# Attention with a two-layer network behind it: when the tiles of h are split, where their halves lie, and which engine splits them

## What is computed

```python
# attention per (batch, head): scores kept where the hash bits of q and k agree
x = attn_out.transpose(0, 2, 1, 3).reshape(B * S, H * D)     # 1536 x 512
h = np.maximum(np.maximum(x @ w1, x @ w2), x @ w3)           # 1536 x 768
y = h @ w_out                                                # 1536 x 512
u = y @ w_in                                                 # 1536 x 2048
g = u * (1.0 / (1.0 + np.exp(-1.702 * u)))
out = g @ w_out2                                             # 1536 x 512
```

## Time and profile before

| | |
|---|---|
| median of 3 runs | 701.23 us (699.51 to 701.7) |
| the profiled execution: device time | 701.48 us |
| its span, first to last instruction | 699.4 us |
| mean granted clock of PE | 0.989 |
| quads, on PE | end at 372.45 us |
| product with w_out, on PE | 372.45 to 430.29 us |
| second network | 430.29 to the end |

### The profile page before, as it was taken

The page is one execution under the profiler, slowest core; times in us unless marked ns, Lnnn a source line. Parts: engine busy times, 40 slices in busy tenths (PEclk is TensorE's granted clock), DMA queues, the critical chain, the costliest instruction groups (busy, mean ns, idle before and its releaser), DMA issues.

```text
span 699.4 us, 11088 instructions
## 1 busy us (share of the span) xinstructions
PE 684.3 (98%) x3970; PEld 596.6 (85%) x3970; DVE 377.2 (54%) x675; ACT 273.9 (39%) x572; POOL 402.9 (58%) x452
## 2 busy tenths in 40 slices
PE   6999999999999999999997999999999999999998
PEld 4777777777767799999996999999999999999996
DVE  6667676767677799768579512322222242222222
ACT  3777777877777530000005113222222232222222
POOL 4755756688876999878738113344444444444441
PEclk9899999999999999999998999999999999999999
DMA  5835736637341110120010101122222141222202
GB/s 119 200 88 137 169 85 152 160 86 177 96 129 62 31 31 30 31 60 25 23 45 1 61 16 45 48 73 62 73 64 61 45 166 61 60 67 69 65 26 90
DMA packets 67141, 54.07 MB, mean 77 GB/s; under 512 B 29200, under 2 KB 56080, under 8 KB 67088
## 3 DMA queue, kind: packets, MB, share of 16 engines
q1 hardware_dynamic: 66768, 53.36, 28.6%
q10 hardware_dynamic: 320, 0.01, 0.0%
HBM read 32.51 MB, written 3.15 MB: 51 GB/s over the span
## 4 chain that ended last, share of the span: by engine, by line
PE 90%; DVE 7%; DMA 1%; issue 1%; SPq 0%; ACTq 0%; ACT 0%; DVEq 0%
PE psS L1017 10%; PE psR L1025 9%; PE psO L1039 9%; PE psR L1087 8%; PE psR L1085 8%; PE psR L1086 8%; PE psS L1085 5%; PE psS L1086 5%; PE psS L1087 5%; PE psS L1188 4%; PE psS L1189 4%; PE psS L1187 4%; DVE probs L856 2%; PE psR L986 2%; PE psO L1188 1%; PE psO L1187 1%
## 5 line engine op out<-in xcount | busy, mean ns | idle before, releaser
L431 POOL TENSOR_SCALAR w_hi<-w_raw 128x512 fp32r<-128x512 f32 (+2 forms) x134 | 84.6, 634 | 189.0 <-PE psO L1189 129.1
L953 DVE TENSOR_TENSOR probs_t<-psR,probs_t 128x384 f32<-128x384 f32 x64 | 35.7, 557 | 181.9 <-ACT probs_t L748 181.9
L456 POOL TENSOR_SCALAR probs<-probs,inv 128x768 f32<-128x768 f32 x96 | 86.4, 909 | 69.1 <-DVE inv L790 68.2
L748 ACT ACTIVATE probs_t<-psR 128x384 f32<-128x384 f32 x64 | 31.5, 492 | 187.9 <-PE psR L1087 187.9
L779 DVE TENSOR_REDUCE neg_max<-psS 128x1 f32<-128x768 f32 x96 | 91.7, 956 | 21.9 <-PE psS L1017 17.6
L565 POOL TENSOR_TENSOR w_lo<-w_raw,w_hi 128x512 fp32r<-128x512 f32 (+1 forms) x68 | 90.8, 1336 | 5.7
L617 ACT ACTIVATE probs<-psS,neg_max 128x768 f32<-128x768 f32 x96 | 86.4, 900 | 11.7 <-DVE neg_max L779 11.7
L1025 PE MATMUL psR<-ident,probs 128*128 128x128 f32 x576 | 75.2, 275 | 0.7 <-DVE bits L774 0.6
L626 ACT ACTIVATE probs_t<-psR 128x384 f32<-128x384 f32 x128 | 59.4, 490 | 35.2 <-PE psR L1025 35.1
L1025 PEld LDWEIGHTS psR<-ident,probs 128*128 128x128 f32 x576 | 67.4, 142 | 4.7 <-issue 2.1
L1039 PE MATMUL psO<-probs_t,v_raw 128*64 128x384 f32 x384 | 68.8, 494 | 0.0
(11 more groups left out here) (197 smaller groups left out, 1544.7 us busy)
## 6 DMA issues: line engine op xcount, KB each, us to landing
w_raw<-in_moe_w_in SPq DMA_DIRECT2D x32, 256.0 KB, 2.7
w_raw<-in_moe_w_out SPq DMA_DIRECT2D x32, 256.0 KB, 2.6
w_raw<-in_moe_w SPq DMA_DIRECT2D x9, 512.0 KB, 3.8
h_lo<-w_hi SPq DMA_DIRECT2D x22, 192.0 KB, 3.4
h_hi<-w_hi SPq DMA_DIRECT2D x18, 192.0 KB, 3.6
w_raw<-in_q SPq DMA_DIRECT2D x16, 192.0 KB, 3.3
w_raw<-in_k SPq DMA_DIRECT2D x16, 192.0 KB, 3.7
v_raw<-in_v SPq DMA_DIRECT2D x16, 192.0 KB, 2.6
```

The source lines that it names most:

```text
L431: return pool.tensor_scalar(dst, src, 1.0, 1.0, ALU.mult, ALU.mult)
L456: pool.tensor_scalar(probs[i % PROBS][:, :], probs[i % PROBS][:, :], inv[:, i % 6:i % 6 + 1], 1.0, ALU.mult, ALU.mult).then_inc(probs_norm ...
```

## The change

1. **Room.** The six arrays `probs` of the attention are given back after use, and `early_h`, of the same size, takes their place. The split halves of batch 0, f = 0, 1, 2 lie there (`EARLY_H` = 3); f = 3, 4, 5 go to `places` 0 to 5, which are free after quad 14. Batch 1 takes `places` 8 to 15 and two chunks of x.
2. **Three tiles early.** ACT copies and DVE subtracts f = 0, 1, 2 of batch 0 behind quad 5, 7 and 11. The DVE instructions stand after all of the quad's own.
3. **The other three by DVE in the last quad.** Six subtractions of 384 columns stand between quad 15's additions; the maxes 1 to 3 come after them. POOL makes no more subtractions for h.
4. **POOL waits.** Split d = 1 of w_out waits for `h_lo_made` 12, the last subtraction of batch 0.
5. **Batch 1 spread.** ACT copies it in halves behind batch 0, each f as soon as its maxes are done. DVE does three of its 12 subtractions ahead of each of the first four `y_lo`, where it did all 12 ahead of the first.
6. PE's order stays; its waits in the tiles 0, 1 and 8 name the new counts.

```diff
-        probs = [sb(f"probs{i}", [P, S], F32) for i in range(PROBS)]
+        with ExitStack() as attention:
+            probs = [attention.enter_context(nc.sbuf_tensor(f"probs{i}", [P, S], F32)) for i in range(PROBS)]
+
+        early_h = sb("early_h", [P, PROBS, S], F32R)
...
+        EARLY_H = 3
+
         def h_part(b, f, lo):
             if b == 0:
-                return places[2 * f + lo]
-            return places[12 + 2 * f + lo] if f < 2 else (x_hi, x_lo)[lo][:, KC + f - 2, :]
+                return early_h[:, 2 * f + lo, :] if f < EARLY_H else places[2 * (f - EARLY_H) + lo]
+            return places[8 + 2 * f + lo] if f < 4 else (x_hi, x_lo)[lo][:, KC + f - 4, :]
...
+        def hidden_done(b, f):
+
+            return h_maxed, 2 * (B * (f - f % 2) + 2 * b + f % 2 + 1)
+
+        def early_after(n):
+
+            return {5: (0,), 7: (1,), 11: (2,)}[n] if n in (5, 7, 11) else ()
...
                 pool.wait_ge(*used(ALL_PARTS - SLOTS + 3 * d + 2))
+                if d == 1:
+                    pool.wait_ge(h_lo_made, 2 * UPS)
                 split(ts(d, S), w_raw[:, k % 3 * BLOCK_COLS:k % 3 * BLOCK_COLS + S], w_hi_made, w_split, ALL_PARTS + d)
-                if d == 0:
-                    for f in range(4):
-                        pool.wait_ge(h_hi_made, f + 1)
-                        pool.tensor_tensor(h_part(0, f, 1), hidden[0][:, f, :, :].rearrange("p j q -> p (j q)"),
-                                           f32(h_part(0, f, 0)), ALU.subtract).then_inc(h_lo_early, 1)
...
             for n in range(QUADS):
                 copy_part(n)
-
-            act.wait_ge(h_maxed, 4 * B * FPS - 4)
+                for f in early_after(n):
+                    if f == 0:
+                        act.wait_ge(*t_split(1, 4))
+                    for j in range(2):
+                        h_hi(0, f, j)
+
             act.wait_ge(quad_made, 7 * (QUADS - 1))
-            for f in range(4):
-                h_hi(0, f)
+            for j in range(2):
+                for f in range(EARLY_H, UPS):
+                    h_hi(0, f, j)
             act.wait_ge(quad_made, 7 * QUADS)
-            for j in range(2):
-                for f in (4, 5):
-                    h_hi(0, f, j)
-            act.wait_ge(h_maxed, 4 * B * FPS)
             for f in range(UPS):
-                h_hi(1, f)
+                for j in range(2):
+                    h_hi(1, f, j)
...
             for n in range(QUADS):
+                last = n == QUADS - 1
                 add_quad(n, 0)
                 add_quad(n, 1)
                 max_quad(n, 0)
+                if last:
+                    for i in range(6, 9):
+                        h_lo(i)
                 add_quad(n, 2)
                 add_quad(n, 3)
+                if last:
+                    for i in range(9, 12):
+                        h_lo(i)
...
+                for f in early_after(n):
+                    h_lo(2 * f)
+                    h_lo(2 * f + 1)
+            for n in range(2 * OUTS):
+                for i in range(3 * n, 3 * n + 3):
+                    if i < 2 * UPS:
+                        h_lo(2 * UPS + i)
+                y_lo(n)
+            for n in range(2 * OUTS, 2 * OUTS * B):
                 y_lo(n)
...
                 if n == 0:
-                    waits = {0: (h_lo_early, 1), 1: (h_lo_early, 2), 2: (h_lo_early, 3), 3: (h_lo_early, 4),
-                             4: (h_lo_made, 1), 5: (h_lo_made, 2)}
+                    waits = {0: (h_lo_made, 6), 3: (h_lo_made, 7), 4: (h_lo_made, 8), 5: (h_lo_made, 9)}
                 elif n == 1:
-                    waits = {4: (h_lo_made, 3), 5: (h_lo_made, 4)}
+                    waits = {3: (h_lo_made, 10), 4: (h_lo_made, 11), 5: (h_lo_made, 12)}
                 elif n == 2 * OUTS:
-                    waits = {f: (h_lo_made, 6 + 2 * f) for f in range(UPS)}
+                    waits = {f: (h_lo_made, 2 * UPS + 2 * f + 2) for f in range(UPS)}
```

More of the change, by code:

```diff
@@ L235, in lsh_attention_ffn @@
         h_lo_made = sem("h_lo_made")
-        h_lo_early = sem("h_lo_early")
         y_ready = sem("y_ready")
@@ L712, in copy_part, with h_hi @@
                 act.activation(quad_parts[n % 2][0], product_bank(7 * n), ACT.Copy).then_inc(part_copied, 1)
[L714 to L717, removed]
+            def h_hi(b, f, j):
+                if j == 0:
+                    act.wait_ge(*hidden_done(b, f))
+                act.activation(h_part(b, f, 0)[:, ts(j, HALF)], hidden[b][:, f, j, :], ACT.Copy).then_inc(h_hi_made, 1)
             for n in range(QUADS):
                 copy_part(n)
-            act.wait_ge(h_maxed, 4 * B * FPS - 4)
+                for f in early_after(n):
[3 more added lines that the diff above has]
+                        h_hi(0, f, j)
             act.wait_ge(quad_made, 7 * (QUADS - 1))
-            for f in range(4):
-                h_hi(0, f)
+            for j in range(2):
+                for f in range(EARLY_H, UPS):
+                    h_hi(0, f, j)
             act.wait_ge(quad_made, 7 * QUADS)
-            for j in range(2):
-                for f in (4, 5):
-                    h_hi(0, f, j)
-            act.wait_ge(h_maxed, 4 * B * FPS)
             for f in range(UPS):
-                h_hi(1, f)
+                for j in range(2):
+                    h_hi(1, f, j)
             def y_hi(n):
@@ L914, in max_quad, with h_lo, y_lo @@
                     mx.then_inc(h_maxed, 1)
-            def h_lo(n, b, f, j):
+            h_order = [(0, f, j) for f in range(EARLY_H) for j in range(2)]
+            h_order += [(0, f, j) for j in range(2) for f in range(EARLY_H, UPS)]
+            h_order += [(1, f, j) for f in range(UPS) for j in range(2)]
+            def h_lo(n):
+                b, f, j = h_order[n]
                 cols = ts(j, HALF)
-                dve.wait_ge(h_hi_made, n)
+                dve.wait_ge(h_hi_made, n + 1)
                 dve.tensor_tensor(h_part(b, f, 1)[:, cols], hidden[b][:, f, j, :], f32(h_part(b, f, 0)[:, cols]),
                                   ALU.subtract).then_inc(h_lo_made, 1)
+            def y_lo(n):
+                b, d, j = n // (2 * OUTS), n // 2 % OUTS, n % 2
+                dve.wait_ge(y_hi_made, n + 1)
+                dve.tensor_tensor(y_part(b, d, 1)[:, ts(j, HALF)], psY[n % len(psY)][:, 0:HALF],
+                                  f32(y_part(b, d, 0)[:, ts(j, HALF)]), ALU.subtract).then_inc(y_lo_made, 1)
             for n in range(QUADS):
+                last = n == QUADS - 1
                 add_quad(n, 0)
@@ L933, in _ @@
                 max_quad(n, 3)
[L934 to L939, removed]
-            def y_lo(n):
-                b, d, j = n // (2 * OUTS), n // 2 % OUTS, n % 2
-                dve.wait_ge(y_hi_made, n + 1)
-                dve.tensor_tensor(y_part(b, d, 1)[:, ts(j, HALF)], psY[n % len(psY)][:, 0:HALF],
-                                  f32(y_part(b, d, 0)[:, ts(j, HALF)]), ALU.subtract).then_inc(y_lo_made, 1)
-            for n in range(2 * OUTS * B):
+                for f in early_after(n):
[7 more added lines that the diff above has]
+            for n in range(2 * OUTS, 2 * OUTS * B):
                 y_lo(n)
```

## The result

The changed kernel takes 692.89 us (median of 4 runs, 692.58 to 693.41) where the kernel before took 701.32 (699.51 to 701.7; four runs, where the table of before has three): a ratio of 0.9886, with a 95% interval of 0.9867 to 0.9904, or 8.4 us less. Measured again beside e9 it was 693.72 against 701.48, ratio 0.9891 [0.9869, 0.9914]. The forecast was 693.8, in a range of 692.2 to 696.4.

A forecast was written before the change was run, and what follows sets the result against it. PE, busy 98% of the span, was taken as the bound, so only its waits or lower clock could be won. In the w_out stage 7.85 us removed less 0.15 put back gives 7.7: 701.48 - 7.7 = 693.8 us, range 692.2 to 696.4.

The forecast's parts named there:

- The last quad and tile 0: Start of the w_out stage: batch 0's last subtraction ends at 374.5, so tile 0's 6.67 us of waits go.
- POOL's wait is hidden: Split d = 1 of w_out, held for h_lo_made 12, is still done 1.0 us before PE's tile 2 wants it.
- The tie at the first y_lo: Tile 4 of w_out: y_lo ends at 384.95, needed at 384.93; 0 to 0.5 us of stall, 0.15 taken.
- The granted clock stays at 1.00: w_out stage: PE no longer pauses, so its clock does not fall and that part of the 1.18 us goes.
- list of losses: w_out stage's 7.92 us lost: 6.67 before tile 1, 1.18 up to tile 4 (clock and first y_lo), 0.07 after.
- The early splits cost nothing: Splits behind quads 5, 7, 11: lag 0.94 to 2.98 us against 1.36 slack at quad 7; none taken, at most 1.6.
- rival B: Early splits of quad 7 press on PE, up to 1.6 us of stall: 695.4 us; chance 0.10.
- The total: Whole kernel: 701.48 less 7.7 gives 693.8 us, range 692.2 to 696.4.
- A: POOL keeps DVE out without turns, PE stalls at tile 3 of w_out, some 2.8 us: 696.4 us; chance 0.07.
- C: No change: DVE's queue is so long that the first y_lo still comes at 392: 701 us; chance 0.03.
- D: DVE becomes the bound of all quads, eight quads with maxes lose 10.4 us: 704.2 us; chance 0.04.

The follow-up runs named there:

- e9: Changed kernel with POOL waiting for h_lo_made 9 and tiles f = 0 and 1 both split behind quad 5, none behind quad 7: 694.16 us, ratio 0.9902.
- e1: Changed kernel without POOL's wait for h_lo_made 12 before split d = 1 of w_out: stage 51.73 us, total 693.73 us.
- e6: Kernel before, with extra matmuls that nobody reads filling PE's waits in tile 0: stage 57.88 us, total 700.99 us, ratio 1.0004.
- e5: Kernel before, with three of batch 1's subtractions ahead of each y_lo, not all 12 ahead of the first: stage 58.42 us, total 700.97 us.
- e2: Changed kernel, but DVE makes all 12 subtractions of batch 1 ahead of the first y_lo: stage 56.62 us, total 699.08 us.
- e3: Changed kernel, but tiles f = 0 and 1 of batch 0 both split behind quad 7, none behind quad 5: stage 50.19 us, total 696.60 us.
- e4: Changed kernel, but the three early tiles all split behind quad 14, not behind quads 5, 7 and 11: stage 52.08 us, total 694.75 us.
- e10: The changed kernel measured again, unchanged: stage 50.18 us, total 693.72 us, ratio 0.9891 to the kernel before.
- e8: Changed kernel with POOL waiting for h_lo_made 9, not 12: stage 49.92 us, total 692.90 us, ratio 0.9893.

## Why the prediction was right, and where not

- **The last quad and tile 0** (6.67 us go): right. The last subtraction of batch 0 ended at 371.56 + 1.49 = 373.05, 2.04 us into the stage with 2.05 forecast.
- **POOL's wait is hidden** by 1.0 us: right. d = 1 was ready at 376.18, wanted at 371.01 + 6.24 = 377.25. e1 shows that leaving it out would have cost 1.6.
- **The tie at the first y_lo**, 0.15 us taken: 0.17 measured. The turns between POOL and DVE held there as in the earlier trace rows: each max and each subtraction took the gap behind one POOL instruction. So close a hit on a tie is in part luck: the prediction had left 0 to 0.5 open, and the next section but one shows that the turns do not always hold.
- **The granted clock stays at 1.00**: right. As the prediction wrote the list of losses, though, 6.67 and 1.18 looked like parts that each could be had alone. They can't: e6 took the clock's part away and gained nothing, since y_lo stood right behind it, and spreading the subtractions alone (e5) gained nothing either. The sum was right because the change removes both. e2 removes the first only and keeps 1.2 of the 7.7 us.
- **The early splits cost nothing**: nearly. The subtractions behind the quads, 5, 7 and 11, and the first and seventh addition of quad 8:

```profile
299.90 1.82 DVE L937 TENSOR_TENSOR early_h<-probs_t,early_h 128x384 fp32r<-128x384 f32 x2
...
316.75 1.76 DVE L937 TENSOR_TENSOR early_h<-probs_t,early_h 128x384 fp32r<-128x384 f32 x2
318.44 0.54 DVE L917 TENSOR_TENSOR v_raw<-psS,early 128x384 f32<-128x384 f32 x1
...
322.43 0.54 DVE L917 TENSOR_TENSOR v_raw<-psS,early 128x384 f32<-128x384 f32 x1
...
343.69 3.42 DVE L937 TENSOR_TENSOR early_h<-probs_t,early_h 128x384 fp32r<-128x384 f32 x2
```

The two behind quad 7 took 1.76, between the 0.94 and 2.98 of the prediction. The quads ran 1.55 us earlier than before up to there (ACT's copy in quad 9 starts at 321.24, before at 322.79), so the first addition of quad 8, at 318.44, is 318.44 - (318.31 - 1.55) = 1.7 us later against PE than it was. That is more than the 1.36 us of slack that the prediction counted, yet at the seventh addition only 0.9 was left of it. The prediction counted one wait of DVE on the way, 0.40; the trace of the kernel before has a second one behind it, 0.48:

```profile
321.69 0.56 DVE L904 TENSOR_TENSOR early<-psR,early 128x384 f32<-128x384 f32 x1 [0.48 <-PE psR L1087]
```

So the slack was 0.40 + 0.48 + 0.96, some 1.8 us. The seventh addition ended at 322.97. PE's product 3 of quad 9 began at 323.06, and its second matmul came 0.25 behind the first, not 0.17:

```profile
323.06 0.41 PE L1111 MATMUL psS<-h_lo,w_hi 128*128 128x384 f32 x1
323.31 0.34 PE L1112 MATMUL psS<-h_lo,w_hi 128*128 128x384 f32 x1
```

From ACT's copy in quad 9 to that in quad 10 it is 7.38 us, 0.1 over. The prediction took 0 and had 1.6 as the upper end; e3 shows what comes behind the edge. What the prediction had not priced here is the clock behind a wait: rival B's 695.4 would have been an underestimate for its own case.
- **The total**, 692.9 for 693.8: 0.9 under, inside the range. The term that is off is the base, as far as the traces tell: the forecast was taken from one profiled execution, whose start was 1.5 us slower than the changed kernel's, and it counted that as part of every run. By the medians it is open, since 701.32 - 692.89 = 8.4 us is 0.7 more than the stage gives, and the interval of the ratio (6.7 to 9.3 us) holds both.
- Rivals A, C and D did not come about. Of A's mechanism something did, though not in the last stage (next section but one).

## What to carry to other kernels

List the waits of a stall in order, and for each ask who comes second: a wait removed shows its worth only when the one behind it is gone too, which one experiment with both and one with each alone tells (0, 0 and 1.6 us here). Where two engines get in each other's way, a wait that keeps one of them still while the other does the urgent work can shorten the whole, as POOL's did by 1.6 us. And price a wait of PE together with the clock that may fall behind it; in e3's profile that doubled it.

## What the runs showed of the hardware

**A wait of PE can cost twice.** Waits that were followed by 1.2 GHz: 1.81 us (e3, 1.84 more), 4.22 (e2, 2.2 more), and the series of waits of the kernel before. In one of e3's four executions, which had a mean clock of 1.000 and took 1.9 us less, the second part seems to have stayed away. Waits that were not: 0.52 (e9), 0.72 and 0.90 (e4), 1.30 (e1), 1.40 (e6). The Trainium skill (page TensorE: Matmul & The Clock Gate, part 1) says that activity holds the clock up and idleness gates it to half; the traces agree in that e6 kept it at 1.00 with matmuls whose results nobody reads.

**DVE can be kept out over several POOL instructions.** Behind quad 11 the first of the two subtractions took 2.95 us of the pair's 3.42 in the table above, and POOL ran on beside it:

```profile
343.35 0.73 POOL L494 TENSOR_TENSOR w_raw<-w_raw 128x256 f32<-128x256 f32 x1
344.05 0.73 POOL L490 TENSOR_TENSOR w_lo<-sum_of_w,w_hi 128x256 fp32r<-128x256 f32 x1
344.75 0.77 POOL L445 TENSOR_SCALAR w_hi<-w_raw 128x256 fp32r<-128x256 f32 x2
345.49 0.73 POOL L490 TENSOR_TENSOR w_lo<-w_raw,w_hi 128x256 fp32r<-128x256 f32 x1
350.46 0.41 POOL L445 TENSOR_SCALAR w_hi<-w_raw 128x256 fp32r<-128x256 f32 x1 [4.24 <-PE psS L1113]
```

At 343.69 DVE's subtraction arrives; POOL's next four instructions keep their undisturbed lengths of 0.40 and 0.73, and only when POOL stops at 346.2 does DVE get through. Behind quad 5, and in e10 behind quad 11, a pair like it took 1.82 or 1.83, with POOL's pieces of 0.73 at 1.05: turns. In the five profiles with the changed kernel's order in the quads (changed, e1, e2, e8, e10) it was 3.4 behind quad 11 in four and 1.83 in one, behind quad 5 1.8 in three and 3.4 in two, and behind quad 7 1.76 in all. The page SBUF — State Buffer of the Trainium skill, section Who interferes with whom, names no turns and says that the order of issue decides who blocks. These rows show that the turns of the earlier trace rows are no rule; but the subtraction here had begun at 343.69 and four POOL instructions that began later passed it, so the order of issue alone doesn't describe them either. What decides between the two is open: the arrival of DVE relative to POOL's instruction is equal to 0.01 us in a case of each kind. In the changed kernel the long form falls where DVE has waits to spare. Had it fallen behind quad 7, its 1.66 us more would have met 0.1 us of slack; no profile shows it there, and how often it falls where can't be said from five.
